# Attention's value products, tail transposes and evictions in another order on TensorE, ScalarE and VectorE

## The reference, cut to what matters

```python
scores = scale * np.matmul(q, k.transpose(0, 1, 3, 2))          # 576 x 576 per head, head_dim 64
thresh = np.max(scores, axis=-1, keepdims=True) - tau
scores = np.where(scores >= thresh, scores, -1000000000.0)
scores = scores - np.max(scores, axis=-1, keepdims=True)
attn = np.exp(scores)
attn = attn / (np.sum(attn, axis=-1, keepdims=True) + 1e-09)
out = np.matmul(attn, v)
```

## Time and profile before

| | |
|---|---|
| median of 3 runs | 826.22 us (826.13 to 826.86) |
| the profiled execution: its time, its span | 826.71 us, 824.9 us |
| attention in it | from about 7 us to 291 us |
| five steps (one pair) in the steady part | 17.09 us |
| PE, DVE, ACT, POOL busy over the span | 99%, 53%, 48%, 49% |

### The profile page before, as it was taken

One profiled execution on the slowest core, in us unless ns is written; L12 is line 12 of the kernel. 1 busy time (PEld: TensorE's weight loads), 2 busy tenths in 40 slices (PEclk: granted clock), 3 DMA queues, 4 the chain that ended last, 5 costly groups with the idle time before them and its releaser, 6 DMA issues.

```text
span 824.9 us, 17529 instructions
## 1 busy us (share of the span) xinstructions
PE 816.9 (99%) x6910; PEld 775.4 (94%) x6910; DVE 438.9 (53%) x995; ACT 396.1 (48%) x1019; POOL 401.4 (49%) x294
## 2 busy tenths in 40 slices
PE   8999999999999999999999999999999999999998
PEld 7989888998889899999999999999999999998986
DVE  6999999999999754422231322313224133366231
ACT  6999999999999843222111221212112112334231
POOL 5999886888775100091370731905508248057000
PEclk9999999999999999999999999999999999999999
DMA  6455444334432022100000000000000102122221
GB/s 157 115 129 127 109 107 115 99 86 111 104 87 69 15 64 78 39 1 29 2 29 1 1 30 1 1 29 2 29 1 1 56 14 93 58 83 96 80 80 64
DMA packets 28624, 49.37 MB, mean 60 GB/s; under 512 B 5440, under 2 KB 14976, under 8 KB 28544
## 3 DMA queue, kind: packets, MB, share of 16 engines
q1 hardware_dynamic: 25728, 43.32, 19.9%
q10 hardware_dynamic: 2816, 4.93, 1.6%
HBM read 38.81 MB, written 8.85 MB: 58 GB/s over the span
## 4 chain that ended last, share of the span: by engine, by line
PE 98%; DVE 1%; issue 0%; DMA 0%; ACT 0%; SPq 0%
PE psum L182 11%; PE psum L811 8%; PE psum L809 8%; PE psum L810 8%; PE psum L825 8%; PE psum L824 8%; PE psum L826 8%; PE psum L340 7%; PE psum L351 7%; PE psum L341 5%; PE psum L1112 2%; PE psum L1113 2%; PE psum L1114 2%; PE psum L1128 2%; PE psum L1127 2%; PE psum L1129 2%
## 5 line engine op out<-in xcount | busy, mean ns | idle before, releaser
L957 DVE SCALAR_TENSOR_TENSOR h_lo<-psum,h_hi 128x288 fp32r<-128x288 f32 x128 | 58.6, 458 | 244.4 <-ACT h_hi L878 244.4
L878 ACT ACTIVATE h_hi<-psum 128x288 fp32r<-128x288 f32 x128 | 52.7, 412 | 255.7 <-PE psum L811 255.7
L809 PE MATMUL psum<-u_split,w_hi 128*128 128x288 f32 x512 | 151.9, 297 | 0.0
L811 PE MATMUL psum<-u_split,w_lo 128*128 128x288 f32 x512 | 151.9, 297 | 0.0
L810 PE MATMUL psum<-u_split,w_hi 128*128 128x288 f32 x512 | 151.6, 296 | 0.0
L1031 POOL TENSOR_TENSOR conv<-x_t,cw 128x576 f32<-128x576 f32 x14 | 16.1, 1151 | 243.5 <-DVE x_t L965 243.0
L586 DVE TENSOR_REDUCE neg_max<-psum 128x1 f32<-128x576 f32 (+1 forms) x160 | 119.2, 745 | 21.0 <-PE psum L341 21.0
L595 DVE SCALAR_TENSOR_TENSOR probs<-psum,thresh,exp_scores 128x576 f32<-128x576 f32 (+1 forms) x160 | 129.2, 808 | 0.0
L437 ACT ACTIVATE exp_scores<-psum,neg_max 128x576 f32<-128x576 f32 (+1 forms) x160 | 118.2, 739 | 0.0
L340 PE MATMUL psum<-qk_split 128*128 128x288 f32 (+1 forms) x320 | 104.5, 342 | 1.4 <-DVE qk_split L574 1.0
L809 PEld LDWEIGHTS psum<-u_split,w_hi 128*128 128x128 f32 x512 | 96.9, 189 | 0.7
(11 more groups left out here) (129 smaller groups left out, 1911.7 us busy)
## 6 DMA issues: line engine op xcount, KB each, us to landing
qk_raw<-in_qk SPq DMA_DIRECT2D x60, 288.0 KB, 4.3
out<-o_sb ACTq DMA_DIRECT2D x18, 256.0 KB, 2.0
v_main<-in_v SPq DMA_DIRECT2D x16, 256.0 KB, 4.5
w_stage<-in_w SPq DMA_DIRECT2D x16, 256.0 KB, 2.7
conv<-in_w SPq DMA_DIRECT2D x16, 256.0 KB, 2.7
conv_dram<-conv SPq DMA_DIRECT2D x7, 576.0 KB, 2.8
gates<-conv_dram SPq DMA_DIRECT2D x7, 576.0 KB, 3.7
w_val_stage<-in_w_val SPq DMA_DIRECT2D x4, 256.0 KB, 3.1
```

The costliest lines, as they stand in the source:

```text
L809: nc.tensor.matmul(out, w1_hi[:, cols], u_hi[:, half, d], start=(d == 0), stop=False)
L811: mm = nc.tensor.matmul(out, w1_lo[:, cols], u_hi[:, half, d], start=False, stop=(d == DB - 1))
```

## The change

Three engines get another order; no instruction is added or removed. On PE, the value products leave the end of the pass, become those of step i-3, and stand behind S1 and ahead of T1. The tails go behind S0. One `weigh_values` that the loop made before stands behind it. On ACT, `evac_main` of the first head is no longer at the end of the pass but in the next one, behind `exponent(2i)`; `evac_main` and `evac_tails` of the second head go behind `exponent(2i+1)`; `spread_inverse` goes behind `guard_sums`. On DVE, `normalise` goes behind `weights(2i)`.

```diff
@@ tensor
             score_rows(2 * i + 1)
             if i < 2:
                 run_warm(4)
+            if i > 2:
+                weigh_values(pe, i - 3)
             if i == STEPS - 1:
                 transpose_tokens(0)
                 transpose_tokens(1)
             if i > 1:
                 transpose_main(i - 2, 1)
-                transpose_tails(pe, i - 2)
             if i + 1 < STEPS:
                 score_rows(2 * i + 2)
             else:
                 transpose_tokens(2)
                 transpose_tokens(3)
+            if i > 1:
+                transpose_tails(pe, i - 2)
             if i > 0:
                 transpose_main(i - 1, 0)
-            if i > 1:
-                weigh_values(pe, i - 2)
-
+
+        weigh_values(pe, STEPS - 3)
         transpose_tokens(4)
         mix_down(0)
@@ scalar
         for i in range(STEPS - 1):
-            if i > 1:
-                spread_inverse(i - 2)
             threshold(2 * i)
             exponent(2 * i)
             if i == 0:
@@
             if i % QB == QB - 1:
                 w1_high(i // QB)
             if i > 1:
+                evac_main(i - 2, 0)
+            if i > 0:
+                guard_sums(i - 1)
+            if i > 1:
+                spread_inverse(i - 2)
+            threshold(2 * i + 1)
+            exponent(2 * i + 1)
+            if i > 1:
                 evac_main(i - 2, 1)
                 evac_tails(act, i - 2)
-            if i > 0:
-                guard_sums(i - 1)
-            threshold(2 * i + 1)
-            exponent(2 * i + 1)
-            if i > 0:
-                evac_main(i - 1, 0)
-
-        spread_inverse(STEPS - 3)
+
         threshold(2 * STEPS - 2)
         exponent(2 * STEPS - 2)
+        evac_main(STEPS - 3, 0)
         guard_sums(STEPS - 2)
+        spread_inverse(STEPS - 3)
         w1_high(PAIRS - 1)
@@ vector
             if i > 0:
                 weights(2 * i - 1)
+            maximum(2 * i + 1)
+            weights(2 * i)
             if i > 2:
                 normalise(dve, i - 3)
-            maximum(2 * i + 1)
-            weights(2 * i)
             if i > 0:
                 reciprocal_sums(i - 1)
```

## The result

The median went from 826.54 to 843.03 us (four runs each, 842.33 to 843.08 after); the ratio is 1.0204, with a 95% interval of 1.0192 to 1.0217. The forecast was 841, from 829 to 849. The profiled execution took 843.08 us with a span of 841.3, against 826.71 and 824.9.

A forecast was written before the change was run, and what follows sets the result against it. The prediction took PE to bound the kernel before, and ACT's chain to hold PE after: 15.2 pairs x 0.97 = +14.7 us, ends +0.4, sum +15.1 on 826.71, forecast 841 us, range 829 to 849.

The forecast's parts named there:

- S1 to W, W to T1, T1 to S0 and T0 to S1: PE's start-to-start times between second-head scores, value products, transposes and next scores: 0.74, 1.24, 0.28 and 0.39 us.
- The link from T0 to S0: PE's time from first-head transposes to the next first-head scores: 2.65 us, or 2.50 in the cast's pass.
- the closed way: Longest dependency loop through a five-step pair over PE, DVE and ACT: 18.06 us, 0.97 above the old 17.09.
- One sign of being wrong: PE's busy time per pair changing by more than 0.25 us would show the switches' cost was forecast wrongly.
- ACT's chain: First-head scores through maximum, thresholds, exponents and evictions to first-head transposes: 4.59 us, 4.41 with 96 columns, 5.10 with `w1_high`.
- The five links: Parts of a pair's longest loop between first-head scores and transposes: 3.40, 2.65, 5.10, 2.50 and 4.41 us.
- all of PE's waiting at T0: PE would wait before first-head transposes: 0.63, 0.48, 0.12 and 0.02 us in passes 4, 1, 2, 3; 1.25 in all.
- ACT's new idle time: ACT's idle time would leave the place before the eviction and turn up before the threshold; no size given.
- Faster at PE's pace: Rival: ACT's chain is shorter than summed, only PE's pace is left; -4.3 us, 822 us; chance 0.08.
- The clock: Rival: PE's idle gaps lower the granted clock for a tenth of attention; 868 us; chance 0.03.
- The tails' wait for `normalise`: Tails held by the later `normalise`: about 0.1 us a step, +8 us upper bound; in a rival of 848 to 855, chance 0.04.
- The ends' +0.4 us: Attention's ends: an early pass loses value products (-0.3 us), the last gains them (+0.7 us); together +0.4 us.

The follow-up runs named there:

- e6: Changed kernel with two small unread activations a pass on ACT between the first exponent and the first eviction; 852.99 us.
- e7: Changed kernel with two small unread activations a pass on ACT between the second eviction and the tails' copy; 843.11 us.
- e1: Changed kernel with the `w1_high` cast moved to the end of its ACT pass, behind the copies; 838.72 us.
- e10: Changed kernel with `spread_inverse` back at the head of ACT's pass; 840.19 us.
- e2: Changed kernel with ACT's second-head eviction ahead of the second head's threshold and exponent; 843.51 us.
- e11: Changed kernel with the value products back at the end of PE's pass and `normalise` back in its old place on DVE; 922.02 us.
- e3: Changed kernel with the tails' transposes again ahead of the first head's scores on PE; 889.03 us.
- e9: Kernel before the change with the `w1_high` cast halved and moved to passes 2 and 3, from the third pair on only; 825.91 us.
- e8: Kernel before the change with the `w1_high` cast made as two halves in passes 2 and 3; 831.84 us.
- e5: Changed kernel with `normalise` back in its old place on DVE, ahead of the second head's maximum; 923.74 us.
- e4: Changed kernel with the value products back at the end of PE's pass, `normalise` staying in its new place; 936.11 us.

## Why the prediction was right

**What bounds the kernel, and what PE pays.** PE was at its pace before, and the new neighbours of W cost nothing that was not forecast: S1 to W, W to T1, T1 to S0 and T0 to S1, read from T0 at 162.87 to S0 at 165.51, took 0.73, 1.24, 0.28 and 0.39 us against 0.74, 1.24, 0.28 and 0.39. The link from T0 to S0, which lies twice in the closed way (2.50 and 2.64 against 2.50 and 2.65), is their sum. One sign of being wrong that the prediction named did show: PE's busy time per pair changed by more than 0.25, from 17.09 to 17.51. It was a poor sign. PE's records overlap (the L340 record of 0.38 us is followed by the next after 0.22), so its busy time counts short waits too; the start-to-start times say that the switches did not get dearer.

**ACT's chain.** The mechanism was right and not only the number. The five links measured 3.46, 2.64, 5.12, 2.50 and 4.43 against 3.40, 2.65, 5.10, 2.50 and 4.41. The extra of a pair was 1.05 where 0.97 was forecast; that difference times 15.2 is 1.2 of the 1.7 us that separate 841.3 from 843.0; the rest is less than what two executions of one kernel differ by. e6 and e7 show it to be the chain and not ACT's load; e1 and e10 shorten it and the time falls.

**What was incomplete.** The forecast put all of PE's waiting at T0, 0.63, 0.48, 0.12 and 0.02 us. Counted from start to start, T0 waits 0.30, 0.27 and 0.19 us in the passes 4, 1 and 2, and T1 waits first in two of them, 0.39 and 0.15 us over the 0.17 that every switch from W shows, for the first eviction: 1.30 in all against 1.25. In the change itself the way over T1 is as long as the one that was forecast (7.82 against 7.81 us by the forecast's links), so leaving it out cost next to nothing. That was luck: with a little more work in the chain (e6) it is the longer one. The same blind spot, the round trip between the two evictions and T1 over one bank, made e2 a miss. ACT's new idle time was forecast ahead of the threshold; the waits show it ahead of the tails' copy (16.2 us in 55), and none ahead of the threshold.

**The rivals.** Faster at PE's pace: no, PE waits. The clock: 1.00 in the pair's stretch, although PE's weight loads now have gaps of 0.2 to 0.6 us several times a pair. Even e11, where PE is idle for about 1.1 us in every pass, shows 1.00 over the 360 us from 20 to 380. The Trainium skill, page "TensorE: Matmul & The Clock Gate", section "A second HAM failure mode: psum-queue depth-cycling", tells of another kernel, in bf16, whose short idle gaps let the clock fall and rise. This kernel does not bear it out: gaps of this size did nothing in 270 us. Nor is the fall at attention's end as certain as the prediction's rows made it look. The same 1.39 us of idle PE stand there in all 13 traces; 0.50 follows in seven, those of before and after among them, and not in the other six (e1, e3, e6, e7, e9, e11). Away from attention's start and end, the one fall in these traces is e8's, behind 3.65 us of idle PE. The tails' wait for `normalise`: it exists (the tails were 0.2 us late in one pass of five, 0.06 after the end of `normalise`) but inside the time that T0 would have waited anyway.

**DVE, transfers, ends.** DVE's busy time per pair stayed (15.99 against 15.81). `normalise` in its old place would have stalled it, as said, by some 80 us (e5). The ends' +0.4 us is not shown: 16.4 less 16.0 is 0.4, but executions of the changed kernel alone lie 0.75 us apart.

## What to carry to other kernels

When three engines in fixed order pass work round through one buffer, write each link as start to start from a trace and add the links along closed ways; an engine with idle time can still set the pace through what stands ahead of the one operation that frees the buffer. Do so for every wait an operation has, the round trip over a shared bank among them, and for the edits meant as a cure too: the ways that I left out (e2, e4) cost more than any link that I mis-sized. Moves that look separate can be one move: the value products, the tails and `normalise` each cost 46 to 93 us when one was put back alone, while the whole costs 16 to 17.

## What was not expected

That the same 0.18 us on ACT costs 9 to 10 us at one place and nothing measurable two microseconds further on. And that a cast moved two passes earlier met a transfer that had been issued 0.1 us before: the data's landing, 3.75 us, was hidden before only because the cast came late. In e8 that wait also took the granted clock to 0.50, a price that gaps of 1 us in every pass (e11) did not have.
